# A fused recurrence, expert attention and spectral mix on one core: scores issued two chunks ahead, the next batch's first clamps moved, the weights' high parts reordered

## The chip, the cores and the metric

The kernel runs on one core of one Trainium2 chip. The metric is device time in microseconds (us) of one execution; lower is better. Before the change the median of three runs is 546.18 us (546.09 to 546.51).

## The reference, cut to what matters

Three layers follow each other, for 4 batches of 768 tokens, all in float32. Only the first and the start of the second lie around the change.

```python
# 1: gated linear recurrence, 8 heads of 48
f = 1.0 / (1.0 + np.exp(-f_logit))
for t in range(S):
    state = f[:, :, t, :, None] * state + np.einsum('bhd,bhe->bhde', k[:, :, t], v[:, :, t])
    y[:, :, t] = np.einsum('bhd,bhde->bhe', q[:, :, t], state)
# 2: x = y with the heads side by side (768 x 384); 4 experts of width 64, the best 2 per token
logits = x @ w_gate
for e in range(E):
    q, k, v = x @ wq[e], x @ wk[e], x @ wv[e]
    a = softmax(where(causal, -1e9, scale * q @ k.T))
    out += mask_e[..., None] * w_e * (a @ v @ wo[e])
# 3: theta = x @ w_theta; x cos(theta), x sin(theta) mixed over tokens by two 768 x 768 matrices,
#    added to x, then u + relu(u @ w_ch)
```

## The kernel before, in words

Every engine has a program of its own, written out by hand, and semaphores tie them together: an instruction waits until a counter has a value, and an engine never passes its own waiting instruction. So the order of calls in the text of each engine is the order on the chip. Batches are 0 to 3; `it` is the batch in the code.

**The gates.** The sigmoid of the gate logits is taken as a logarithm, `ln(1 + exp(-x))`: VectorE clamps one head pair (`clamp_gates`, L969), ScalarE takes Exp (L598) and Ln (L603), VectorE scans (`scan`, L975), ScalarE makes the decays from the scan (L607, L622, L627), and GpSimd scales q and k with them (L529, L532). This is done for batch b+1 while batch b is worked on. For batch 0 it is done first thing, in three parts of 256 tokens.

**The recurrence** is computed in 6 chunks c of 128 tokens. In a chunk TensorE has four blocks of work:

- scores of chunk c (`scores`, L1403): k times q of 8 heads, 16 weight loads, on 64 x 128 parts of the array, two row halves in turn; into one of two PSUM buffers, c % 2;
- turn_k (L1458): k of a chunk turned for the state's increment, on 64 x 128 parts too, 8 loads and products 48 wide;
- increments (L1476): turned k times v, on 128 x 64 parts, 16 loads, products 48 wide;
- outputs (L1495 with the masked scores, L1501 with the state): on 128 x 32 parts, 56 loads, products 128 wide.

VectorE masks the scores (`mask`, L1103; its output Am shares memory with `probT` and is shown under that name), which needs scores(c) and, as Am has two buffers, the outputs of chunk c-2. Then it adds the increment to the state (L1121) and decays it (L1125). ScalarE copies the turned k (L765) and the outputs (L776, L777). In the order before, chunk c of TensorE's loop is scores(c+1), turn_k(c+1), increments(c), outputs(c). VectorE's loop is mask(c+1), then the state of c.

**The ring.** When VectorE has made the low part of x for chunk n (`x_low`, L1044; ScalarE made the high part), TensorE multiplies x by the value and gate weights (6 products, n = 0 to 5), then by the query and key weights (8 products), each as high*high + high*low + low*high (L1385 to L1387). VectorE copies the values out (L1180), computes the routing (L1200 to L1220) and makes the low parts of q and k (`qk_l`, L1241). The query and key products need the low parts of their weights, which in batch 0 GpSimd makes (L535), once all of x's low parts and all four clamps are done.

**The attention.** TensorE's first expert scores (L1545) stand in front of the last two ring products and wait for the fourth `qk_l`. From there, VectorE's maxima (L1230), ScalarE's exponentials (L834) and TensorE's transposes (L1450) and products (L1608) hand work to each other. Layer 3 (4 batches after all four of layer 2) follows; it is nearly all TensorE.

The code below has the waits of each.

Of the kernel before, what the change touches and what calls it, by code (L numbers as in the profile page):

```python
# [26 lines left out]
NT = T // P  # L27
# [194 lines left out]
def build(nc, fT, qT, kT, vT, v, wq, wk, wv, w_gate, wo, woT, w_theta, w_tok, w_ch, out, slow_x):  # L222
    with ExitStack() as ctx:
# [268 lines left out]
        def _(pool):  # L492
# [46 lines left out]
            pool.wait_ge(w_hi, 1)  # L539
# [54 lines left out]
        def _(act):  # L594
# [152 lines left out]
            for it in range(B):  # L747
# [11 lines left out]
                def recurrence_copies():  # L759
                    for c in range(NT):  # L760
# [17 lines left out]
                        if it < 1:  # L778
                            if c == 2:
                                grow_first(2)  # L780
                            elif c == 3:
                                act.wait_ge(w_in[0], 32)
                                hi(wqk_h[:, :, :], staged(W_QK, 1536), w_hi)
                                act.wait_ge(w_in[1], 32)
                                hi(wvg_h[:, :, 0:256], wv_raw, w_hi)
                                hi(wvg_h[:, :, 256:260], graw[:, :, :], w_hi)
                            elif c == NT - 2:
                                for n in range(NT - 2):
                                    x_high(n)
                            elif c == NT - 1:  # L790
                                x_high(NT - 2)
                                exp_gates(1, (0, 1))
# [44 lines left out]
                for n in range(FIRST_QK, RING):  # L837
                    if n == FIRST_QK:
# [5 lines left out]
                        if it < 1:  # L844
                            log_gates(1, (0, 1))
                            exp_gates(1, (2, 3))
                            log_gates(1, (2, 3))
                            grow(1, 0)
                        elif it < B - 1:
                            if it == 1:  # L850
                                late_weights()
                            grow(it + 1, 1)
# [104 lines left out]
        def _(dve):  # L957
# [139 lines left out]
            for it in range(B):  # L1097
# [13 lines left out]
                for c in range(NT - 1):  # L1111
# [17 lines left out]
                    if it < 1:  # L1129
# [6 lines left out]
                        elif c == NT - 3:  # L1136
                            clamp_gates(1, 0)
                            clamp_gates(1, 1)
                        elif c == NT - 2:
                            dve.wait_ge(w_hi, 3)  # L1140
# [34 lines left out]
                if it < 1:  # L1175
                    clamp_gates(1, 2)
                    clamp_gates(1, 3)
# [204 lines left out]
        def _(pe):  # L1382
# [63 lines left out]
            for it in range(B):  # L1446
# [70 lines left out]
                for c in range(1, NT):  # L1517
                    if it < 1 and c == 2:
                        pe.wait_ge(v_in, 16)
                    if c + 1 < NT:  # L1520
                        scores(it, c + 1)
                        if c + 2 < NT:
                            turn_k(c + 1)
                        increments(c)
                    outputs(c)
# [255 lines left out]
```

## Time and profile before

| what | value |
|---|---|
| median of three runs | 546.18 us |
| the profiled execution's own time | 545.76 us |
| its span, first to last instruction | 544.0 us |
| TensorE matmul busy | 520.8 us (96%) |
| TensorE weight load busy | 487.3 us (90%) |
| VectorE busy | 384.8 us (71%) |
| ScalarE busy | 286.0 us (53%) |
| GpSimd busy | 133.7 us (25%) |
| granted TensorE clock | full in all 40 slices |

The time is read against the span: 1.8 us of the execution's own time lie outside it. PE is TensorE's products and PEld its weight loads; for the small products of the recurrence the loads are the better clock, since a load's start is recorded and the end of a product is modelled. A bracket at a row's end gives the idle time in front of it and what ended it; "issue" means that nothing the profile shows ended it. The three stretches of recurrence of batches 1 to 3 lie at 92, 162.6 and 233 us, that of batch 0 at 14.8 to 39.6 us.

### The profile page before, as it was taken

The numbers are of one execution on the slowest core, as the hardware profiler recorded it, in microseconds if no ns is written. First come the engines' busy times: TensorE is split into PE (matmuls) and PEld (weight loads), VectorE is DVE, ScalarE is ACT, GpSimd is POOL, SyncE is SP. The second block draws the span as 40 slices with busy tenths as digits, with TensorE's granted clock in tenths as the row PEclk, the third lists the DMA queues.
The fourth block names the chain that finished last, engine by engine and source line by source line (L and its number), as shares of the span: only waits on it lengthen the run. The fifth ranks groups of instructions, "written<-read, shape, count | busy, mean of one in ns | idle before, by whom it ended". The sixth has DMA issues, their size and how long they took to land.

```text
span 544.0 us, 14180 instructions
## 1 busy us (share of the span) xinstructions
PE 520.8 (96%) x6012; PEld 487.3 (90%) x6012; DVE 384.8 (71%) x698; ACT 286.0 (53%) x591; POOL 133.7 (25%) x89
## 2 busy tenths in 40 slices
PE   3999999999999999999999999999999999999997
PEld 1679778997889988899978899999999999999997
DVE  5989988898797977765877698585347654574434
ACT  5767687656976459642587574343234333333311
POOL 2005064065500054100214257112211212022110
PEclk9999999999999999999999999999999999999999
DMA  8958022072210620003500000311030201220032
GB/s 279 339 195 332 1 61 61 4 284 82 60 30 4 220 118 2 2 4 132 220 1 2 1 2 0 88 46 43 1 82 20 74 0 40 51 87 1 0 88 87
DMA packets 24832, 42.74 MB, mean 79 GB/s; under 512 B 3264, under 2 KB 15552, under 8 KB 24384
## 3 DMA queue, kind: packets, MB, share of 16 engines
q1 hardware_dynamic: 24768, 41.83, 23.5%
q8 instruction: 47, 0.77, 0.6%
q14 instruction: 17, 0.14, 0.1%
HBM read 32.25 MB, written 4.72 MB: 68 GB/s over the span
## 4 chain that ended last, share of the span: by engine, by line
PE 81%; DVE 7%; ACT 7%; issue 2%; DMA 1%; SPq 1%; DVEq 0%; ACTq 0%
PE bank L1385 18%; PE bank L1387 18%; PE bank L1386 18%; PE bank L1403 5%; ACT prob L834 5%; PE bank L1608 5%; PE bank L1545 4%; PE bank L1495 4%; PE bank L1450 2%; PE bank L1501 2%; PE bank L1476 2%; DVE nmax L1230 1%; DVE gate L975 1%; DMA OT<-w_theta 1%; DVE probT L1250 1%
## 5 line engine op out<-in xcount | busy, mean ns | idle before, releaser
L1385 PE MATMUL bank<-wt_h,z_h 128*128 128x384 f32 x288 | 97.0, 337 | 0.0
L1387 PE MATMUL bank<-wt_h,z_l 128*128 128x384 f32 x288 | 96.7, 336 | 0.0
L1386 PE MATMUL bank<-wt_l,z_h 128*128 128x384 f32 x288 | 96.4, 335 | 0.0
L834 ACT ACTIVATE prob<-bank,nmax 128x384 f32<-128x384 f32 (+5 forms) x96 | 60.3, 638 | 21.1 <-DVE nmax L1230 21.1
L589 POOL TENSOR_TENSOR trig<-trig,x 128x768 f32<-128x768 f32 x18 | 33.5, 1860 | 142.3 <-ACT trig L708 142.3
L1230 DVE TENSOR_REDUCE nmax<-bank 128x1 f32<-128x384 f32 (+5 forms) x96 | 54.9, 616 | 10.3 <-PE bank L1551 5.2
L1059 DVE TENSOR_SCALAR turns<-bank 128x384 int32<-128x384 f32 x22 | 12.2, 554 | 68.1 <-PE bank L1387 68.1
L1385 PEld LDWEIGHTS bank<-wt_h,z_h 128*128 128x128 f32 x288 | 54.0, 188 | 0.3 <-issue 0.3
L1387 PEld LDWEIGHTS bank<-wt_h,z_l 128*128 128x128 f32 x288 | 54.1, 188 | 0.0
L1386 PEld LDWEIGHTS bank<-wt_l,z_h 128*128 128x128 f32 x288 | 54.0, 187 | 0.0
L1608 PE MATMUL bank<-probT,Vm 128*64 128x128 f32 x672 | 42.0, 276 | 0.7 <-DVE probT L1250 0.2
L700 ACT COPY x<-bank 128x384 f32<-128x384 f32 x24 | 11.5, 478 | 55.2 <-PE bank L1387 55.2
L1608 PEld LDWEIGHTS bank<-probT,Vm 128*64 128x64 f32 x672 | 36.2, 137 | 2.9 <-DVE probT L1250 1.4
L1103 DVE TENSOR_TENSOR probT<-bank,keep 128x1024 f32<-128x1024 f32 x24 | 29.3, 1221 | 10.8 <-PE bank L1403 10.7
L1495 PE MATMUL bank<-probT,V 128*32 128x128 f32 x768 | 35.8, 275 | 0.7 <-issue 0.7
L1545 PE MATMUL bank<-qk_h 64*128 64x512 f32 (+3 forms) x128 | 26.2, 407 | 7.6 <-ACT prob L834 5.8
L705 ACT ACTIVATE trig<-r 128x384 f32<-128x384 f32 x22 | 11.6, 527 | 41.6 <-DVE r L1071 41.6
L1385 PE MATMUL bank<-xT_h,wqk_h 128*128 128x384 f32 x96 | 32.9, 343 | 0.0
L1386 PE MATMUL bank<-xT_l,wqk_h 128*128 128x384 f32 x96 | 32.4, 338 | 0.0
L1387 PE MATMUL bank<-xT_h,wqk_l 128*128 128x384 f32 x96 | 32.4, 337 | 0.0
L1250 DVE COPY probT<-bank 128x896 f32<-128x896 f32 x24 | 26.0, 1085 | 7.8 <-PE bank L1450 7.8
L1403 PE MATMUL bank<-q,k 64*128 64x128 f32 x384 | 29.8, 291 | 1.4 <-issue 1.4
(179 smaller groups left out, 1371.9 us busy)
## 6 DMA issues: line engine op xcount, KB each, us to landing
gate<-fT SPq DMA_DIRECT2D x12, 384.0 KB, 3.2
q<-qT SPq DMA_DIRECT2D x12, 384.0 KB, 5.4
k<-kT SPq DMA_DIRECT2D x12, 384.0 KB, 6.3
wt_raw<-w_tok SPq DMA_DIRECT2D x6, 768.0 KB, 8.8
uT<-xb SPq DMA_DIRECT2D x64, 72.0 KB, 2.1
out<-uT SPq DMA_DIRECT2D x24, 192.0 KB, 2.3
V<-v SPq DMA_DIRECT2D x3, 1344.0 KB, 11.1
gate<-fT SPq DMA_DIRECT2D x3, 512.0 KB, 5.6
```

Of the source, the lines that this page charges most:

```text
L589: nc.gpsimd.tensor_tensor(trig[:, s % 2, :, :], trig[:, s % 2, :, :], x2[:, s:s + 1, :].broadcast_to([P, 2, D]), ALU.mult).then_inc(z_made, 1)
L834: nc.scalar.activation(prob[:, m % 2, r, at], bank[r][:, at], ACT.Exp, bias=nmax[:, m, k:k + 1], accum_out=den[:, m // 2, which, e:e + 1]) ...
L1103: nc.vector.tensor_tensor(Am[:, c % 2, :, :], bank[c % 2][:, :].rearrange("p (h t) -> p h t", h=H), keep[:, None, :].broadcast_to([P, H, P ...
L1230: nc.vector.tensor_reduce(nmax[:, m, k:k + 1], bank[r][:, columns_of(m, which)], X, ALU.max, negate=True).then_inc(max_done, 1)
L1250: nc.vector.tensor_copy(probT[:, m % 2, 1, :].rearrange("p (c h q) -> p h c q", h=2, q=64), turned(m, 1)).then_inc(pt_copied[0], 1)
L1385: nc.tensor.matmul(o, a_h, b_h, start=start, stop=False)
L1386: nc.tensor.matmul(o, a_h, b_l, start=False, stop=False)
L1387: return nc.tensor.matmul(o, a_l, b_h, start=False, stop=stop)
L1403: mm = nc.tensor.matmul(bank[c % 2][:, slot(h):slot(h) + P], k[r:r + 64, h // 2, at], q[r:r + 64, h // 2, at], start=True, stop=True)
L1495: mm = nc.tensor.matmul(dst, V[:, c, at:at + BLOCK], Am[:, c % 2, slot(h) // P, :], start=n == 0, stop=c == 0 and n + 1 == len(parts), ski ...
L1545: mm = nc.tensor.matmul(bank[r][:, lo_:hi_], x[rows, a, queries], y[rows, 2 + a, keys], start=fresh_bank and n == 0, stop=False, skip_grou ...
L1608: mm = nc.tensor.matmul(ps(values_bank(m))[64 * r:64 * r + 64, at], Vm[:, s, e * ED:(e + 1) * ED], probT[:, m % 2, r, n * P:(n + 1) * P], ...
```

## The change

It has four parts. (1) TensorE: in the recurrence the scores run two chunks ahead: the chunk loop becomes turn_k(c+1), increments(c), scores(c+2), outputs(c), with scores(2) still in front at c = 1. In batch 0 scores(4) stays behind the outputs of chunk 2, since its q and k are scaled late. (2) VectorE: the clamps of batch 1 for pairs 0 and 1 leave the recurrence of batch 0 (c = 3), those for pairs 2 and 3 leave the place behind the low parts, and all four now stand behind x_low(1) to x_low(4). (3) ScalarE: the exponentials of batch 1's pairs 0 and 1 leave the last chunk of batch 0's recurrence and stand after it. (4) ScalarE makes the high part of the query and key weights after those of the value weights; the counts of `w_hi` that others wait for follow.

```diff
-            pool.wait_ge(w_hi, 1)
+            pool.wait_ge(w_hi, 3)
...
                                 act.wait_ge(w_in[0], 32)
-                                hi(wqk_h[:, :, :], staged(W_QK, 1536), w_hi)
                                 act.wait_ge(w_in[1], 32)
                                 hi(wvg_h[:, :, 0:256], wv_raw, w_hi)
                                 hi(wvg_h[:, :, 256:260], graw[:, :, :], w_hi)
+                                hi(wqk_h[:, :, :], staged(W_QK, 1536), w_hi)
...
                             elif c == NT - 1:
                                 x_high(NT - 2)
-                                exp_gates(1, (0, 1))
...
                         if it < 1:
-                            log_gates(1, (0, 1))
-                            exp_gates(1, (2, 3))
-                            log_gates(1, (2, 3))
+                            for pairs in ((0, 1), (2, 3)):
+                                exp_gates(1, pairs)
+                                log_gates(1, pairs)
                             grow(1, 0)
...
-                        elif c == NT - 3:
-                            clamp_gates(1, 0)
-                            clamp_gates(1, 1)
                         elif c == NT - 2:
-                            dve.wait_ge(w_hi, 3)
+                            dve.wait_ge(w_hi, 2)
...
                 for n in range(NT):
                     x_low(n)
-                if it < 1:
-                    clamp_gates(1, 2)
-                    clamp_gates(1, 3)
+                    if it < 1 and 1 <= n < NT - 1:
+                        clamp_gates(1, n - 1)
...
+                    late = it < 1 and c + 2 == NT - 2
                     if c + 1 < NT:
-                        scores(it, c + 1)
+                        if c == 1 or it < 1 and c + 1 == NT - 2:
+                            scores(it, c + 1)
                         if c + 2 < NT:
                             turn_k(c + 1)
                         increments(c)
+                        if c + 2 < NT and not late:
+                            scores(it, c + 2)
                     outputs(c)
```

Above that loop the changed file drops comment lines, so its numbers are 5 lower: its scores are L1398, turn_k L1453, increments L1471, outputs L1490 and L1496.

This is how TensorE's program stands in batch 1, from the scores of chunk 3 to the outputs of chunk 3 (before). Each row is one block; the outputs of a chunk are some 14 rows, of which the first two stand here.

```order
L1403 MATMUL bank<-q,k 128x128 x8
L1458 MATMUL bank<-ident,k 128x48 x8
L1476 MATMUL bank<-V,kTs 48x48 x8
L1495 MATMUL bank<-probT,V 32x128 x4
L1501 MATMUL bank<-q,S 32x128
...
L1403 MATMUL bank<-q,k 128x128 x8
L1458 MATMUL bank<-ident,k 128x48 x8
L1476 MATMUL bank<-V,kTs 48x48 x8
L1495 MATMUL bank<-probT,V 32x128 x4
```

The same place in the changed program, from the increments of chunk 1 on:

```order
L1471 MATMUL bank<-V,kTs 48x48 x8
L1398 MATMUL bank<-q,k 128x128 x8
L1490 MATMUL bank<-probT,V 32x128 x4
L1496 MATMUL bank<-q,S 32x128
...
L1453 MATMUL bank<-ident,k 128x48 x8
L1471 MATMUL bank<-V,kTs 48x48 x8
L1398 MATMUL bank<-q,k 128x128 x8
L1490 MATMUL bank<-probT,V 32x128 x4
```

The scores, which stood between outputs and turn_k, now stand between increments and outputs. The number of instructions is the same.

VectorE in batch 0, from the first low part of x on, before:

```order
L1044 TENSOR_TENSOR xT_l<-xt,xT_h 128x3x128 x6
L969 TENSOR_SCALAR gate<-gate,floor 128x768 x2
L1180 COPY Vm<-bank 128x260 x4
L975 SCALAR_TENSOR_TENSOR gate<-fresh,gate 128x768
L1180 COPY Vm<-bank 128x260
```

and in the changed program:

```order
L1043 TENSOR_TENSOR xT_l<-xt,xT_h 128x3x128 x2
L968 TENSOR_SCALAR gate<-gate,floor 128x768
L1043 TENSOR_TENSOR xT_l<-xt,xT_h 128x3x128
L968 TENSOR_SCALAR gate<-gate,floor 128x768
L1043 TENSOR_TENSOR xT_l<-xt,xT_h 128x3x128
L968 TENSOR_SCALAR gate<-gate,floor 128x768
L1043 TENSOR_TENSOR xT_l<-xt,xT_h 128x3x128
L968 TENSOR_SCALAR gate<-gate,floor 128x768
L1043 TENSOR_TENSOR xT_l<-xt,xT_h 128x3x128
L1175 COPY Vm<-bank 128x260 x4
```

Four clamps now stand between the first low part and the first copy of values, where two stood; the other two came from the recurrence, ahead of this piece.

## Rows read from the trace of the kernel before

**Rows 1.** Stages: busy time of each engine in batch 1's recurrence.
```profile
core 0: us, PE busy (x) PEld busy (x) DVE busy (x) ACT busy (x) POOL busy (x), PEclk, DMA share, GB/s
92.00:110.50 18.50, 18.50 (x516) 16.66 (x512) 15.35 (x24) 12.89 (x25) 0.38 (x1) 1.00 0.02 6
```

**Rows 2.** Timeline, TensorE's weight loads, batch 1 (start, us, instruction, [idle before]).
```profile
98.64 0.97 PEld L1403 LDWEIGHTS bank<-q,k 64*128 64x128 f32 x16 [0.20 <-issue]
99.52 0.39 PEld L1458 LDWEIGHTS bank<-ident,k 48*128 48x128 f32 x8
99.96 0.44 PEld L1476 LDWEIGHTS bank<-V,kTs 128*48 128x48 f32 x16
100.46 0.16 PEld L1495 LDWEIGHTS bank<-probT,V 128*32 128x32 f32 x8
...
102.12 0.97 PEld L1403 LDWEIGHTS bank<-q,k 64*128 64x128 f32 x16 [0.20 <-issue]
...
105.61 0.97 PEld L1403 LDWEIGHTS bank<-q,k 64*128 64x128 f32 x16 [0.20 <-issue]
106.70 0.44 PEld L1476 LDWEIGHTS bank<-V,kTs 128*48 128x48 f32 x16
...
109.15 0.11 PEld L1501 LDWEIGHTS bank<-q,S 128*32 128x32 f32 x1 [0.27 <-DVE S L1125]
...
110.60 0.19 PEld L1385 LDWEIGHTS bank<-wvg_h,xT_h 128*128 128x128 f32 x1 [0.20 <-issue]
```

**Rows 3.** Timeline, VectorE, end of batch 1's recurrence.
```profile
106.82 1.23 DVE L1103 TENSOR_TENSOR probT<-bank,keep 128x1024 f32<-128x1024 f32 x1 [1.14 <-PE bank L1403]
...
109.89 2.88 DVE L1044 TENSOR_TENSOR xT_l<-xt,xT_h 128x384 fp32r<-128x384 f32 x6
```

**Rows 4.** The chain that ended last, after batch 1's recurrence.
```profile
110.33 2.42 DVE xT_l L1044 x5
```

**Rows 5.** Timeline, TensorE's weight loads, batch 0.
```profile
27.34 0.37 PEld L1458 LDWEIGHTS bank<-ident,k 48*128 48x128 f32 x8 [1.61 <-issue]
27.76 0.44 PEld L1476 LDWEIGHTS bank<-V,kTs 128*48 128x48 f32 x16
...
31.75 0.14 PEld L1495 LDWEIGHTS bank<-probT,V 128*32 128x32 f32 x5
32.85 0.11 PEld L1495 LDWEIGHTS bank<-probT,V 128*32 128x32 f32 x2 [0.96 <-issue]
...
34.50 0.97 PEld L1403 LDWEIGHTS bank<-q,k 64*128 64x128 f32 x16 [0.20 <-issue]
35.60 0.44 PEld L1476 LDWEIGHTS bank<-V,kTs 128*48 128x48 f32 x16
...
39.89 0.19 PEld L1385 LDWEIGHTS bank<-wvg_h,xT_h 128*128 128x128 f32 x1 [0.59 <-issue]
```

**Rows 6.** DMA queues from 24 to 33 us: packets, MB, share of 16 engines.
```profile
q8 instruction: 2, 0.03, 1.4%
```

**Rows 7.** Timeline, VectorE, batch 0.
```profile
33.88 0.62 DVE L969 TENSOR_SCALAR gate<-gate,floor 128x768 f32<-128x768 f32 x1 [0.47 <-DMA gate<-fT]
...
35.72 1.23 DVE L1103 TENSOR_TENSOR probT<-bank,keep 128x1024 f32<-128x1024 f32 x1 [0.19 <-PE bank L1403]
...
39.22 2.90 DVE L1044 TENSOR_TENSOR xT_l<-xt,xT_h 128x384 fp32r<-128x384 f32 x6 [0.28 <-ACT xT_h L757]
42.04 1.14 DVE L969 TENSOR_SCALAR gate<-gate,floor 128x768 f32<-128x768 f32 x2
...
44.55 0.43 DVE L1180 COPY Vm<-bank 128x260 f32<-128x260 f32 x1 [0.36 <-PE bank L1387]
44.90 2.09 DVE L975 TENSOR_TENSOR_SCAN gate<-fresh,gate 128x768 f32<-128x768 f32 x1
...
53.61 2.41 DVE L1241 SCALAR_TENSOR_TENSOR qk_l<-bank,qk_h 128x384 fp32r<-128x384 f32 x5
```

**Rows 8.** Timeline, GpSimd and ScalarE, batch 0.
```profile
38.83 1.57 ACT L598 ACTIVATE gate<-gate 128x768 f32<-128x768 f32 x2
...
43.37 6.85 POOL L535 TENSOR_TENSOR wqk_l<-OT,wqk_h 128x384 fp32r<-128x384 f32 x4 [14.45 <-DVE gate L969]
```

**Rows 9.** Timeline, TensorE's weight loads, first expert scores of batch 0.
```profile
56.11 0.19 PEld L1545 LDWEIGHTS bank<-qk_h 64*128 64x128 f32 x2 [0.25 <-DVE qk_l L1241]
```

## The prediction

> **What bounds the kernel now.** I read the page first: TensorE is busy nearly all the time, so a change pays only where TensorE waits or where its own work gets shorter. Then the stages: in batch 1's recurrence its products cover 18.50 of 18.50 us [rows 1]. Busy is not yet full speed, so I went to the weight loads in order of time [rows 2], where the reader should look at starts. From the scores of one chunk (98.64) to those of the next (102.12) it is 3.48 us: scores to turn_k 0.88, turn_k to increments 0.44, increments to outputs 0.50, outputs to scores 1.66. In none of these is there a wait for another engine. The only one in the whole recurrence is 0.27 us for the last state [rows 2]. Batches 2 and 3 show the same starts to 0.02 us. So what the change wants to take off the path, the wait of outputs for masked scores, is not there in three batches of four.
>
> Behind a recurrence the chain that ended last goes through VectorE's low parts and its backlog [rows 4]. VectorE itself idles 1.14 us before its last mask, waiting for scores(5), and is then busy up to the low parts [rows 3]. So it starts later whenever TensorE's recurrence ends later, and nothing swallows the delay.
>
> Batch 0 differs. There are two pauses of TensorE, 1.61 and 0.96 us, that no engine explains [rows 5]. Counted in TensorE's program they stand exactly 256 instructions apart, and in the same stretch the queue that carries instructions moved two packets [rows 6], while the 16 DMA engines were full of inputs. I take both as instructions that came late: then they belong to a place in the stream, not to a piece of work. At the end of that recurrence TensorE waits 0.59 us for VectorE [rows 5].
>
> **Part 1, scores ahead, batches 1 to 3.** All work is kept; what changes is the neighbours. Scores and turn_k use the array in the same 64 x 128 parts, and turn_k's loads start 0.88 us after the scores', before their last load is done. Where scores are followed by another shape, increments after scores(5), it is 1.09 us (105.61 to 106.70) [rows 2]. In the new order all three moved blocks are followed by outputs, another shape (128 x 32). I take 1.09 for each. Per batch two of them lose the cheap neighbour: 2 x (1.09 - 0.88) = +0.42. Increments before scores I price as increments before outputs, 0.50, and outputs before turn_k as outputs before scores, 1.66; these stay. A turn_k that starts afresh took 0.42 to the increments in batch 0 (27.34 to 27.76) [rows 5] against 0.44: -0.04 for two. **Per batch +0.38, for three batches +1.14 us.** Bounds: nothing, if outputs can follow scores as turn_k does; 0.15 more per block, if scores idle as long behind increments as behind outputs (0.44 of loads and 0.20 [rows 2], 0.64 against 0.50), for nine blocks.
>
> The 0.27 us wait stays. Before, mask(5) starts when scores(5) end, just as increments(4) begin (106.70, 106.82) [rows 2, 3]. After, mask(5) has its scores early but still needs the outputs of chunk 3, whose last product again ends as increments(4) begin. Mask, sum and decay then race the same outputs(4).
>
> The Trainium skill (TensorEngine Tiling (Array Packing), Key Properties) says that changing the tiling mode drains TensorE, and it speaks against this change, which turns three changes of shape per chunk into four. This trace agrees where products 128 wide are in flight (0.20, and 1.09 against 0.88) and not where they are 48 wide: turn_k to increments shows no idle time. By the page, every change drains, scores behind increments too; that is the upper bound above, and the sum would be 9 x 0.15 = 1.35 us higher.
>
> **Part 1, batch 0.** Only scores(3) and scores(5) move. The first pause lies one instruction before the end of scores(3). In the new stream that place is just behind the last product of outputs(1), so the outputs are counted as done before it, and VectorE's and ScalarE's work on q and k for chunk 4 keeps its time. I leave it at 1.61. Everything before the second pause again fits in front of 32.85. Before, 51 of 56 loads of outputs(3), then all of scores(5) lay between the pause and increments(4): 32.85 to 35.60 [rows 5]. After, the pause falls after 6 of the 16 loads of scores(5). What remains is some 0.7 us of them and 1.67 of outputs(3): 32.85 + 0.7 + 1.67 = 35.2. So 0.40 us are won, since scores use the time of the pause. mask(5) (35.72) moves to 35.3, and with it the first low part (39.22 to 38.8) and the ring (39.89 to 39.5) [rows 5, 7].
>
> The Trainium skill (Runtime: NRT & Kernel Launch, Instruction fetch mechanics) says instructions are refilled in blocks of 16 KiB, 256 instructions, with a cost that is "mostly hidden". The 256 agree with this trace; "hidden" does not hold in batch 0, where 1.61 and 0.96 us show. Were it hidden and the pauses due to the work, the sum would lose the 0.40.
>
> **Part 2, the clamps.** In the old place two of them cost nothing: VectorE waited around them (33.88) [rows 7]. In the new place VectorE has no slack: from 39.22 to the fifth `qk_l` it idles once, 0.36 us before the fourth copy [rows 7]. Two clamps are 1.14 less 0.08 of overlap, 1.06 us. Starting 0.40 earlier, filling the 0.36: 1.06 - 0.40 - 0.36 = **+0.30** for everything from the scan at 44.90 on. Who waits? Low part n gets behind by up to three clamps, 1.6 us, but the ring takes about 1.1 us a product and a low part 0.47, so x_low(n) still lands some 0.8 us early. GpSimd starts behind the last low part instead of the last clamp: 38.8 + 2.8 + 2.1 + 0.2 = 43.9 or 44.0 against 43.37 [rows 8], 1.71 us a part, first part at 45.7, second at 47.4; TensorE wants them at 39.5 + 6.6 = 46.1 and 1.6 later, 47.7. Thin, 0.3 us, but covered. The first expert scores want the fourth `qk_l`: 53.61 + 0.57 + 3 x 0.46 = 55.56, after 55.86, seen by TensorE at 55.92. TensorE itself would be there at 56.11 - 0.40 = 55.71 [rows 9]. **So 0.19 us of the 0.40 come through.** What follows is a chain of all three engines, and moves as one.
>
> **Parts 3 and 4.** ScalarE's two exponentials (1.57 us) [rows 8] leave the front of the last copy of x and wait for the new clamps, done at 40.4 and 41.4; two more activations of 0.8 and the first logarithm is there at 43.0, the scan needs it at 45.2. The value weights' high part comes 1.5 us earlier, but VectorE takes it behind the last state either way. Both nothing; if ScalarE were 2.2 us later it would show in the scan one to one.
>
> **Sum** against the profiled execution's 545.76: +1.14 - 0.19 = +0.95, 546.7. The median of the runs lies 0.42 above that execution: 546.18 + 0.95 = **547.1 us**. A measurement of this kernel tells about 0.2%, 1.09 us, from no change, so this sits just inside it.
>
> **The rivals.**
>
> - *Shape is free (546.0, chance 0.17).* Outputs follow scores as cheaply as turn_k does; then only batch 0's -0.19 is left. For: 128 x 32 parts could be loaded one by one. Against: the only change of shape after scores, 106.70, costs the 0.21.
> - *VectorE or GpSimd late in batch 0 (547.9, 0.16).* The clamps among the low parts delay the ring, or GpSimd's parts miss TensorE by a few tenths, or the second pause grows and the 0.40 is lost: +1.14 + 0.6. For: margins of 0.3 us. It decides from 0.15 us of extra delay on, when the sum passes 1.09.
> - *Every change drains (548.5, 0.07).* Scores behind increments idle a full 0.20: 0.64 - 0.50 = 0.14 to 0.15 in nine blocks, 1.35 on top of 547.1. Against: increments to outputs, also a change, shows 0.50 with 0.44 of loads.
> - *The gaps are waits (faster, about 544.0, 0.10).* The 0.20 before each scores block is the wait for the mask and not a drain. Then moving scores behind increments hides it: nine blocks and two in batch 0, 11 x 0.20 = 2.2 us off, and no 0.21 added: 546.2 - 2.2. It decides for faster once 0.10 of the 0.20 is such a wait and the 0.21 falls away. Against: the same 0.20 stands before the ring at 110.60, where no scores are involved [rows 2].
>
> **How the numbers follow.** My forecast has 0.50, its own range is 546.7 to 547.6: about 0.31 of it below 547.27 and 0.19 above. Faster 0.11 (the last rival and 0.01 of a larger gain in batch 0). Slower: 0.19 + 0.16 + 0.07, less a little where the late rival stays small: 0.41. Same: 0.48. The range 545.4 to 548.1 holds the forecast, the free shape and the late rival, and leaves the two outer ones.
>
> **What would show it.** Scores to outputs at 1.09 us in the loads of batches 1 to 3, and recurrences 0.4 us longer from first scores to ring. The 0.27 wait still there. In batch 0 a pause inside scores(5) after six loads, increments(4) near 35.2, the ring near 39.5, the first `qk_l` at 53.9, expert scores at 55.9. I am wrong if scores to outputs takes 0.9, if the pauses sit elsewhere or have other lengths, or if the ring of batch 0 shows gaps.

## The result: 2.3 us slower

| what | before | changed |
|---|---|---|
| median of the runs | 546.10 us (545.51 to 546.51, 6 runs) | 548.42 us (548.12 to 548.93, 6 runs) |
| ratio to before, 95% interval | | 1.0046 (1.0033 to 1.0059) |
| span of the profiled execution | 544.0 us | 546.4 us |

The change makes the kernel slower by 0.46%, more than the 0.2% that a measurement tells from no change. The forecast was 547.1, its range ended at 548.1, and the time lies 0.3 us above that.

The first place to look is where the difference builds up. These are the starts of the ring and of the first expert scores in each batch, read from TensorE's weight loads in both traces:

| batch | ring before | ring changed | difference | expert scores before | changed | difference |
|---|---|---|---|---|---|---|
| 0 | 39.89 | 39.47 | -0.42 | 56.11 | 56.24 | +0.13 |
| 1 | 110.60 | 111.48 | +0.88 | 126.84 | 127.69 | +0.85 |
| 2 | 181.13 | 182.76 | +1.63 | 197.36 | 198.97 | +1.61 |
| 3 | 251.66 | 254.01 | +2.35 | 272.04 | 274.39 | +2.35 |

So each recurrence of batches 1 to 3 is 0.72 to 0.74 us longer (the forecast had 0.38), batch 0 gives +0.15 at its end (forecast -0.19), and nothing behind the last recurrence adds or takes anything. 3 x 0.73 + 0.15 = 2.34 us, which is the difference of the last row and, to 0.1, that of the spans. These are two single executions. Where batch 0 begins differs between executions (see the experiments), so its row is worth less than the other three.

TensorE's weight loads in batch 1 of the changed kernel (start, us, instruction, idle before), to be laid beside [rows 2]:

```profile
103.51 0.33 PEld L1453 LDWEIGHTS bank<-ident,k 48*128 48x128 f32 x8 [0.20 <-issue]
103.89 0.44 PEld L1471 LDWEIGHTS bank<-V,kTs 128*48 128x48 f32 x16
104.39 0.97 PEld L1398 LDWEIGHTS bank<-q,k 64*128 64x128 f32 x16
105.48 0.16 PEld L1490 LDWEIGHTS bank<-probT,V 128*32 128x32 f32 x8
...
107.14 0.44 PEld L1471 LDWEIGHTS bank<-V,kTs 128*48 128x48 f32 x16 [0.20 <-issue]
108.25 0.19 PEld L1490 LDWEIGHTS bank<-probT,V 128*32 128x32 f32 x8 [0.67 <-issue]
...
111.48 0.19 PEld L1380 LDWEIGHTS bank<-wvg_h,xT_h 128*128 128x128 f32 x1 [0.20 <-issue]
```

Scores (104.39) to outputs (105.48) is the 1.09 of the forecast, turn_k afresh to increments 0.38 where it had 0.42. The new thing is 0.67 us of idle loads before outputs(4), and the 0.27 before the last state is gone. The row says "issue", so it names nobody. The chain that ended last does, in the same place (start, us, what):

```profile
107.28 0.48 ACT xT_h L776
107.76 0.39 ACT xt L777
108.15 0.14 issue
108.29 0.43 PE bank L1490 x8
```

The path leaves TensorE here for ScalarE's two copies of the outputs of chunk 3. The cost groups of the page say it for the whole program (busy, mean ns, idle before and its releaser):

```profile
L1490 PE MATMUL bank<-probT,V 128*32 128x128 f32 x768 | 35.1, 275 | 2.3 <-ACT xt L777 1.9
L1490 PEld LDWEIGHTS bank<-probT,V 128*32 128x32 f32 x768 | 29.1, 109 | 4.6 <-issue 2.5
```

ScalarE's own timeline shows that the copies themselves are prompt, as they were before. First the changed kernel, then the same two copies in the kernel before, where outputs(4) began only at 107.19:

```profile
107.28 0.48 ACT L776 CAST xT_h<-bank 128x384 fp32r<-128x384 f32 x1 [1.66 <-PE bank L1496]
107.66 0.48 ACT L777 COPY xt<-bank 128x384 f32<-128x384 f32 x1
```

```profile
105.75 0.48 ACT L776 CAST xT_h<-bank 128x384 fp32r<-128x384 f32 x1 [1.51 <-PE bank L1501]
106.12 0.48 ACT L777 COPY xt<-bank 128x384 f32<-128x384 f32 x1
```

Outputs of chunks 1 to 4 all go to PSUM bank 4 (`out_bank`), so outputs(4) wait until both copies of outputs(3) are out. That is 1.1 us after outputs(3) have ended and increments(4) begun (107.14 to 108.25). Before, scores(5) and increments(4) stood between the two outputs, 1.09 + 0.49 = 1.58 us. Now only the increments do, 0.49.

Batch 0 shows the same wait with one copy instead of two. There ScalarE makes the high part later, so only L777 stands between outputs(3) and outputs(4), and these begin 0.73 us after the increments (35.08 to 35.81 in the rows of batch 0 below).

The sum of one recurrence, from the loads of both traces: two scores blocks at 1.09 instead of 0.89, +0.40; two turn_k at 0.38 instead of 0.44, -0.12; increments(4) to outputs(4) 1.11 instead of 0.49, +0.62; outputs(4) and (5) 3.23 instead of 3.41, -0.18, since the state is now in time. Together +0.72.

Batch 0, TensorE's loads, to be laid beside [rows 5]:

```profile
27.02 0.35 PEld L1453 LDWEIGHTS bank<-ident,k 48*128 48x128 f32 x8 [1.75 <-issue]
...
31.41 0.52 PEld L1398 LDWEIGHTS bank<-q,k 64*128 64x128 f32 x6
32.55 0.74 PEld L1398 LDWEIGHTS bank<-q,k 64*128 64x128 f32 x10 [0.63 <-issue]
...
35.08 0.44 PEld L1471 LDWEIGHTS bank<-V,kTs 128*48 128x48 f32 x16 [0.20 <-issue]
35.81 0.19 PEld L1490 LDWEIGHTS bank<-probT,V 128*32 128x32 f32 x8 [0.29 <-issue]
...
37.32 0.11 PEld L1490 LDWEIGHTS bank<-probT,V 128*32 128x32 f32 x2 [0.24 <-issue]
...
39.47 0.19 PEld L1380 LDWEIGHTS bank<-wvg_h,xT_h 128*128 128x128 f32 x1 [0.26 <-issue]
...
56.24 0.19 PEld L1545 LDWEIGHTS bank<-qk_h 64*128 64x128 f32 x2 [0.80 <-DVE qk_l L1236]
```

The first pause stands behind outputs(1), the second inside scores(5) after six loads. There is a small third one, 44 loads into outputs(4), again 256 instructions on. Neither this pause nor the wait for the copy reaches the ring. It starts 0.11 us after the first low part of x is finished (38.80 + 0.56 to 39.47), as it did before (39.22 + 0.56 to 39.89). VectorE in the same batch, to be laid beside [rows 7]:

```profile
35.29 1.23 DVE L1102 TENSOR_TENSOR probT<-bank,keep 128x1024 f32<-128x1024 f32 x1 [2.15 <-PE bank L1496]
...
38.80 1.03 DVE L1043 TENSOR_TENSOR xT_l<-xt,xT_h 128x384 fp32r<-128x384 f32 x2 [0.27 <-ACT xt L777]
...
43.74 1.43 DVE L1175 COPY Vm<-bank 128x260 f32<-128x260 f32 x4
45.08 2.51 DVE L974 TENSOR_TENSOR_SCAN gate<-fresh,gate 128x768 f32<-128x768 f32 x1
47.52 0.40 DVE L1175 COPY Vm<-bank 128x260 f32<-128x260 f32 x1
47.84 2.19 DVE L974 TENSOR_TENSOR_SCAN gate<-fresh,gate 128x768 f32<-128x768 f32 x1
```

The first scan starts 0.12 before its forecast of 45.2 but takes 2.51 us, where it took 2.09. GpSimd, beside [rows 8]:

```profile
43.98 6.86 POOL L535 TENSOR_TENSOR wqk_l<-OT,wqk_h 128x384 fp32r<-128x384 f32 x4 [15.46 <-DVE xT_l L1043]
```

### The profile page after: what moved, and what is told of

The parts are those of the page before. It is cut to its first block, busy times and chain, and to the rows that moved or that the text cites. A ratio compares the mean times of both kernels' runs of the same rounds, so it can differ in the third digit from the quotient of the medians.

```text
span 546.4 us, 14181 instructions
## 1 busy us (share of the span) xinstructions
PE 519.6 (95%) x6012; PEld 486.9 (89%) x6012; DVE 385.3 (71%) x698; ACT 285.6 (52%) x591; POOL 133.8 (24%) x89
## 4 chain that ended last, share of the span: by engine, by line
PE 76%; DVE 11%; ACT 9%; issue 2%; DMA 1%; DVEq 0%
PE bank L1380 18%; PE bank L1382 17%; PE bank L1381 17%; ACT prob L833 5%; PE bank L1608 5%; PE bank L1398 4%; PE bank L1545 4%; PE bank L1490 4%; DVE gate L974 2%; PE bank L1445 2%; PE bank L1496 2%; PE bank L1471 1%; DVE nmax L1225 1%; DVE qk_l L1236 1%; DVE probT L1245 1%
## 5 line engine op out<-in xcount | busy, mean ns | idle before, releaser
L1490 PE MATMUL bank<-probT,V 128*32 128x128 f32 x768 | 35.1, 275 | 2.3 <-ACT xt L777 1.9
L1490 PEld LDWEIGHTS bank<-probT,V 128*32 128x32 f32 x768 | 29.1, 109 | 4.6 <-issue 2.5
```

The lines of the kernel that those rows point to most:

```text
L1490: mm = nc.tensor.matmul(dst, V[:, c, at:at + BLOCK], Am[:, c % 2, slot(h) // P, :], start=n == 0, stop=c == 0 and n + 1 == len(parts), ski ...
```

## The experiments

Before's median was 545.83, 545.64 and 545.81 us in the three sessions. "Ring" and "expert scores" below are starts in the trace, as differences to the trace of before. The start of an execution moves: in the kernels whose TensorE program is the same up to the first pause, that pause ends between 26.85 us (`clamps_back`) and 28.14 us (`first_only`). So batch 0 is judged by differences inside one trace.

### Each half alone

`scores_only` is the kernel before with the new order of scores and nothing else; `rest_only` is the changed kernel with the old order.

```diff
 # scores_only, against the kernel before
+                    late = it < 1 and c + 2 == NT - 2
                     if c + 1 < NT:
-                        scores(it, c + 1)
+                        if c == 1 or it < 1 and c + 1 == NT - 2:
+                            scores(it, c + 1)
...
                         increments(c)
+                        if c + 2 < NT and not late:
+                            scores(it, c + 2)
```

> The kernel before with the new order of scores alone (clamps, exponentials and weights' high parts as before). Theory A, from the trace of the changed kernel: in each of batches 1 to 3 outputs(4) waits about 0.67 us for ScalarE's copy of outputs(3), since scores(5) no longer stand between them, and the recurrence is 0.72 us longer; batch 0 wins the 0.4 us in front of its ring and keeps it, because no clamp was moved into VectorE's backlog. Sum: +3 x 0.72 - 0.4 = +1.8 us on the kernel before, about 547.9. Rival: the loss belongs to the clamps and VectorE's backlog in batch 0 and the new order is harmless: at most +0.4 us.

> The changed kernel with the old order of scores (so the clamps among the low parts, the exponentials behind the recurrence and the new order of weights' high parts are left). Theory A: batches 1 to 3 keep their 3.48 us per chunk and the single wait of 0.27 us; in batch 0 VectorE's backlog grows by two clamps less one idle 0.36 us, 0.7 us, and the fourth low part of q and k comes at about 56.3 to 56.6 us instead of 55.6, so the expert scores start 0.2 to 0.5 us late: +0.2 to +0.5 us, about 546.5. Rival: these parts carry the loss: +2 us. Rival: they cost nothing: 0.

`scores_only`: 548.31 us, ratio 1.0047 (1.0034 to 1.006). Recurrences +0.71 to +0.74 each, 0.67 before outputs(4), ring and expert scores of batch 0 both 0.33 earlier. `rest_only`: 546.16 us, ratio 1.0004 (0.9995 to 1.0012). Its recurrences keep 3.48 us a chunk and the 0.27 wait; its ring is 0.32 earlier, of which 0.25 are there when the first pause ends, its expert scores 0.23 later. So the recurrences of batches 1 to 3 make all that the measured times can tell, and the other parts cost some half a microsecond between the ring and the expert scores of batch 0.

The half microsecond is seen in traces alone. `scores_only` has a median 2.48 us above before, more than its three recurrences (2.2 us) and more than the 1.8 us that was expected with a gain in batch 0; its profiled execution, 547.58 us, was its fastest. By the medians it can't be told from the changed kernel.

### A bank of its own for outputs(4)

```diff
-    return 6 if c == NT - 1 else 4
+    return 6 if c == NT - 1 else 7 if c == NT - 2 else 4
...
-                    if 1 <= c < NT - 1:
+                    if 1 <= c < NT - 2:
```

The ring's product that uses bank 7 next waits for the copy of outputs(4) in its place.

> The changed kernel with outputs(4) written to a PSUM bank of their own (the one that the turned k of odd heads has left), so that they need not wait for the copy of outputs(3); the ring's fifth product, which uses that bank later, waits for the copy instead. Theory A: the 0.67 us wait of outputs(4) goes, the 0.27 us wait for the last state comes back, so each of batches 1 to 3 is 0.42 us shorter, and batch 0 stays: -1.3 us on the changed kernel, about 547.1. Rival: the wait was for something else (the mask, or instructions), and nothing changes.

547.36 us, ratio 1.0027 (1.0017 to 1.0037). Batch 1's loads:

```profile
107.03 0.44 PEld L1471 LDWEIGHTS bank<-V,kTs 128*48 128x48 f32 x16 [0.20 <-issue]
109.57 0.11 PEld L1496 LDWEIGHTS bank<-q,S 128*32 128x32 f32 x1 [0.36 <-DVE S L1124]
111.02 0.19 PEld L1380 LDWEIGHTS bank<-wvg_h,xT_h 128*128 128x128 f32 x1 [0.20 <-issue]
```

The wait before outputs(4) is gone and the one for the state is back. From first scores to ring a recurrence takes 18.91 us against 18.53 before, +0.38 in each of the three batches, which is the forecast's 0.38; from ring to ring a batch adds 0.35. In batch 0 the increments are again followed by outputs(4) after 0.50 us (35.04 to 35.54). With a bank of their own for outputs(4) half of each recurrence's loss goes: the wait for the copy is shown to be that half.

### Scores(5) back behind the outputs

```diff
-                    late = it < 1 and c + 2 == NT - 2
+                    ahead_by_two = c + 2 < NT - 1 and not (it < 1 and c + 2 == NT - 2)
...
-                        if c == 1 or it < 1 and c + 1 == NT - 2:
+                        if c == 1 or it < 1 and c + 1 == NT - 2 or c + 1 == NT - 1:
                             scores(it, c + 1)
...
-                        if c + 2 < NT and not late:
+                        if ahead_by_two:
```

> The changed kernel with scores(5) back in front of increments(4); scores(3), and from batch 1 on scores(4), stay ahead. Theory A: scores(5) again cover ScalarE's copy of outputs(3), the 0.67 us wait goes and 0.27 us for the state comes back: each of batches 1 to 3 is 0.42 us shorter, as with a bank of its own; batch 0 loses the 0.4 us that scores(5) won inside the pause for instructions, of which VectorE's backlog lets none through, or makes them late by as much: -0.9 to -1.3 us on the changed kernel, 547.1 to 547.5. Rival: each block of scores ahead costs the same and the last is not special: -0.3 us at most.

547.86 us, ratio 1.0036 (1.0023 to 1.0049), and 0.53 to 0.57 a batch. The expectation missed: the wait moved one chunk up instead of going.

```profile
104.94 0.19 PEld L1490 LDWEIGHTS bank<-probT,V 128*32 128x32 f32 x8 [0.29 <-issue]
...
110.18 0.11 PEld L1496 LDWEIGHTS bank<-q,S 128*32 128x32 f32 x1 [0.27 <-DVE S L1124]
```

Now outputs(3) have only turn_k(4) and increments(3) between them and outputs(2), 0.38 + 0.49 = 0.87 us where the copies need 1.11. So 0.24 is waited for, and the sum comes out again: +0.40 - 0.12 + 0.24 = 0.52, where a recurrence measures 19.08 to 19.09 us against 18.53. Whatever stands between two outputs has to cover the copies of the first.

### Keeping turn_k behind the scores

From c = 2 on the order is increments(c), scores(c+2), turn_k(c+1), outputs(c), with the bank of `own_bank`. Scores still run two chunks ahead, but their neighbour is the block of their own shape.

> The changed kernel with outputs(4) in a bank of their own, and turn_k put behind the scores in each chunk: chunk 1 is scores(2), scores(3), turn_k(2), increments(1), outputs(1), later ones are increments(c), scores(c+2), turn_k(c+1), outputs(c). Scores stay two chunks ahead, but every block of them is followed by a block on the same 64 x 128 parts. Theory A (what the move of scores costs, besides the copy wait, is the change of shape behind them): scores to turn_k 0.88 us again, turn_k to outputs 0.44, so a chunk takes 3.48 us as before and the recurrence of batches 1 to 3 is 0.0 to 0.2 us shorter than before; 1.1 us less than the changed kernel with its own bank alone, about 546.2. Rival (being ahead costs by itself, through PSUM or the masks): no better than that kernel, 547.3.

545.77 us, ratio 1.0000 (0.9991 to 1.0009).

```profile
100.33 0.97 PEld L1398 LDWEIGHTS bank<-q,k 64*128 64x128 f32 x16
101.22 0.38 PEld L1453 LDWEIGHTS bank<-ident,k 48*128 48x128 f32 x8
101.65 0.16 PEld L1490 LDWEIGHTS bank<-probT,V 128*32 128x32 f32 x8
...
103.32 0.44 PEld L1471 LDWEIGHTS bank<-V,kTs 128*48 128x48 f32 x16 [0.20 <-issue]
```

Scores to turn_k is 0.89 again, turn_k to outputs 0.43, and one recurrence is 18.43 us against 18.53 before. The 0.20 after the outputs stays and now stands before the increments: it belongs to leaving the products 128 wide, whoever follows. So both terms of the loss are removed by construction, the price of the neighbour by order and the copy by bank, and scores two chunks ahead are worth 0.1 us a recurrence by themselves in these batches, which the times can't tell from nothing.

### Only batch 0 ahead

```diff
+                    late = it < 1 and c + 2 == NT - 2
...
-                        scores(it, c + 1)
+                        if it >= 1 or c == 1 or c + 1 == NT - 2:
+                            scores(it, c + 1)
...
+                        if it < 1 and c + 2 < NT and not late:
+                            scores(it, c + 2)
```

> The kernel before with scores(3) and scores(5) ahead in batch 0 alone; clamps and all else as before. Theory A: scores(5) run inside the second pause for instructions, the ring of batch 0 and its expert scores start 0.3 to 0.4 us earlier, and everything behind moves by that: -0.35 us on the kernel before, 545.5 to 545.8. Rival (the gain is lost in VectorE's backlog): expert scores at 56.1 us as before, no difference.

545.96 us, ratio 1.0004 (0.9995 to 1.0013). In its trace ring and expert scores are 0.28 later, not earlier. The first pause ended 0.8 later, at 28.14 against 27.34; from there to the ring it is 12.04 us against 12.55. This is not the expected gain seen: the second pause is missing altogether in this trace, where TensorE came late to it, while `scores_only`, with the same order in batch 0 and a first pause that ended at 26.96, takes 12.60 us for the same stretch. The differences between executions are larger than the gain, and the times don't show it. Inconclusive.

### GpSimd earlier

`rest_only`, with GpSimd's low parts of the query and key weights waiting for the high parts alone:

```diff
             pool.wait_ge(w_hi, 3)
-            pool.wait_ge(x_lo, NT)
-            pool.wait_ge(clamped, gates(1, PAIRS))
```

> The changed kernel with the old order of scores (as in an earlier run), and GpSimd's low parts of the query and key weights no longer held until the low parts of x: they start when the high parts are made, at about 33 us. Theory B (VectorE's first two scans after the ring's start take 2.5 and 2.2 us instead of 1.75 because GpSimd subtracts beside them): both scans take 1.75 us, the fourth low part of q and k comes 1.1 us earlier, and the expert scores start at or before 55.8 us: -0.4 to -0.5 us on that run in the trace, if the masks of the recurrence, which now have GpSimd beside them, do not get longer. Rival: the scans stay at 2.2 to 2.5 us; the cause is another (reading the values' banks, ScalarE's logarithms).

547.58 us, ratio 1.0026 (0.9996 to 1.0056). The interval is wide and just takes in no change; the trace has its expert scores of batch 0 2.18 us later than before. It was to be faster and is not, but it tells what slows the scans. VectorE:

```profile
39.79 1.83 DVE L1041 TENSOR_TENSOR xT_l<-xt,xT_h 128x384 fp32r<-128x384 f32 x2
41.54 1.37 DVE L966 TENSOR_SCALAR gate<-gate,floor 128x768 f32<-128x768 f32 x1
42.84 1.35 DVE L1041 TENSOR_TENSOR xT_l<-xt,xT_h 128x384 fp32r<-128x384 f32 x1
44.11 0.61 DVE L966 TENSOR_SCALAR gate<-gate,floor 128x768 f32<-128x768 f32 x1
44.64 0.55 DVE L1041 TENSOR_TENSOR xT_l<-xt,xT_h 128x384 fp32r<-128x384 f32 x1
...
48.45 1.74 DVE L972 TENSOR_TENSOR_SCAN gate<-fresh,gate 128x768 f32<-128x768 f32 x1
```

and GpSimd beside it:

```profile
38.53 5.24 POOL L535 TENSOR_TENSOR wqk_l<-OT,wqk_h 128x384 fp32r<-128x384 f32 x4 [9.47 <-issue]
```

While GpSimd works (to 43.77) the second and the third low part take 1.36 and 1.35 us instead of 0.55 and a clamp 1.37 instead of 0.61; once it is done the scan takes 1.74 instead of 2.09 to 2.51. The collision had only been moved onto the low parts, which the ring waits for one by one: its loads idle 1.04 us before the first product and 1.43 until the third low part is there.

### The state before the mask

The kernel before with two blocks exchanged in the last step of a recurrence: TensorE does increments(4), scores(5), outputs(4), and VectorE takes the last state before the last mask.

> The kernel before with one change, in the last step of each recurrence: TensorE does increments(4), scores(5), outputs(4) instead of scores(5), increments(4), outputs(4), and VectorE adds and decays the last state before it masks scores(5) instead of behind it. Theory A: the 0.27 us wait for the last state is a race of mask, sum and decay (2.3 us) against increments(4) and outputs(4); with the state done while scores(5) run, only the mask is left behind them and outputs(5) find both ready. Each recurrence is 0.27 us shorter and VectorE gets to the low parts 0.5 us earlier: -0.8 to -1.5 us on the kernel before, about 545.0. Rival: outputs(5) then wait for the mask as long as they did for the state: no difference.

545.25 us, ratio 0.9990 (0.9981 to 1.0000). The recurrence of batch 1 is 18.45 us against 18.53, with 0.20 before outputs(5) in place of the 0.27. That is 0.08 where 0.27 was expected; the rival, that outputs(5) then wait for the mask instead, is most of the truth.

```profile
108.08 0.16 PEld L1498 LDWEIGHTS bank<-probT,V 128*32 128x32 f32 x8 [0.20 <-DVE probT L1103]
```

The rest of its 1.0 us of span (543.0) was there when batch 0 ended (its ring is 0.76 earlier), so most of it may be one execution's luck. It is the fastest version tried, and still inside the 0.2%.

### The clamps back, twice

`clamps_back` is the changed kernel, and `turn_no_clamps` the kernel `turn_behind`, each with the clamps and exponentials of batch 1 in their old places.

```diff
+                        elif c == NT - 3:
+                            clamp_gates(1, 0)
+                            clamp_gates(1, 1)
...
-                    if it < 1 and 1 <= n < NT - 1:
-                        clamp_gates(1, n - 1)
+                if it < 1:
+                    clamp_gates(1, 2)
+                    clamp_gates(1, 3)
```

> The changed kernel with the clamps and exponentials of batch 1 back in their old places, and nothing else undone. If part 2 costs some 0.5 us between ring and first expert scores of batch 0, these come at about 55.75 instead of 56.24 with the ring where it was (39.5), batches 1 to 3 keep their 0.72 to 0.74 us each, and the whole is 0.5 us below the changed kernel: ratio to before 1.0034 (1.0025 to 1.0045). If part 2 costs nothing, the ratio stays at 1.0046.

> The changed kernel with outputs(4) in a bank of its own, turn_k between scores and outputs, and the clamps and exponentials of batch 1 back in their old places. If the clamps among the low parts cost through VectorE's backlog and the longer first scan (0.3 to 0.5 us of batch 0), the first scan takes 2.1 to 2.25 us instead of 2.51, the first expert scores come 0.3 us earlier than in the kernel before (0.5 earlier than with the clamps moved), and the whole is 0.3 to 0.6 us below the kernel before: ratio 0.9990 (0.998 to 1.000). If the clamps cost nothing and the 0.3 us come from the order of TensorE, the expert scores stay 0.2 to 0.3 us late and the ratio is 1.0000.

`clamps_back`: 548.24 us, ratio 1.0043 (1.003 to 1.0057). `turn_no_clamps`: 545.67 us, ratio 0.9994 (0.9985 to 1.0003). From ring to expert scores both take 16.2 us, as before; the changed kernel, `rest_only`, `own_bank` and `turn_behind`, with the clamps among the low parts, take 16.75 to 16.77 (`last_late`, whose ring started 0.7 later, 16.43). This half of the expectation came true to 0.05 us. Both kernels also have ScalarE's exponentials back, so parts 2 and 3 are not told apart. Part 4 is still in both. But in `clamps_back` the ring started at 39.91 and not at 39.5, for the third late block of instructions, 0.24 in the changed kernel, was 1.34 us here:

```profile
34.49 0.44 PEld L1476 LDWEIGHTS bank<-V,kTs 128*48 128x48 f32 x16 [0.20 <-issue]
...
37.82 0.11 PEld L1495 LDWEIGHTS bank<-probT,V 128*32 128x32 f32 x2 [1.34 <-issue]
...
39.91 0.19 PEld L1385 LDWEIGHTS bank<-wvg_h,xT_h 128*128 128x128 f32 x1 [0.20 <-issue]
...
56.12 0.19 PEld L1550 LDWEIGHTS bank<-qk_h 64*128 64x128 f32 x2 [0.25 <-DVE qk_l L1241]
```

TensorE reached increments(4) 1.1 us before the kernel before did and then stood at the place of the next block. What batch 0 wins ahead of a block of instructions, the next block can take back. The ratio of 1.0034 that was expected was not met; its interval holds both that and the changed kernel's 1.0046, so the medians do not show what the clamps cost. Nor do they in `turn_no_clamps`, whose expert scores came 0.14 us later than before and not 0.3 earlier.

### Both small gains together

The kernel before, with the scores of batch 0 ahead (as `first_only`) and the end of `state_first` in batches 1 to 3.

> The kernel before with two orders: in batch 0 the scores run ahead as in the change, in batches 1 to 3 the last step is increments(4), scores(5), outputs(4), and VectorE takes the last state ahead of the last mask. The parts add: 0.3 to 0.4 us from the ring of batch 0, since scores(5) use the time of the second pause, and 0.08 in each later batch, in which a wait of 0.2 before outputs(5) is left of the 0.27 for the state. Ratio 0.9989 (0.998 to 1.000). If the ring's gain in batch 0 is taken up before the first expert scores, as it may be with VectorE's row of work behind it, 0.9996.

545.76 us, ratio 0.9999 (0.999 to 1.0008). The expert scores of batch 0 are 0.12 earlier, and each later batch adds 0.06 to 0.08, in all 0.33 us of span. The later batches are as expected; batch 0 gave a third of what was hoped, and less than its first pause ended early (27.17 against 27.34). The whole can't be told from no change.

## Why the prediction missed, step by step

**Part 1, batches 1 to 3, the price of the neighbour: right.** 1.09 where 1.09 was forecast; `own_bank` isolates it at +0.35 a batch, and `turn_behind` takes it away. That every change of shape drains is refuted: increments to scores is 0.50 in every trace (103.89 to 104.39). A free shape is refuted by the 1.09, and gaps that are waits for the mask by the 0.20, which stays behind the outputs and now stands before turn_k or the increments.

**"Increments before scores I price as increments before outputs, 0.50 ... Mask, sum and decay then race the same outputs(4)": the step that failed.** Increments(4) to outputs(4) stayed at 0.50 in the sum and measured 1.11. The step followed VectorE's race for the outputs and left out ScalarE's. Outputs(4) need the bank that outputs(3) filled, so they wait for two copies, which are done 1.1 us after outputs(3). Scores(5) had hidden that. The term missing from the sum is 0.62 for the wait less 0.18 that the state no longer costs, 0.44 a batch, less 0.08 because turn_k afresh was cheaper than taken. Three batches: 3 x 0.35 = 1.05 us. The 0.27 wait "stays" was wrong for the same reason. It would have stayed had the outputs not been late, as in `own_bank`, where it is 0.36.

**Part 1, batch 0: the places right, the 0.40 by luck.** The pauses are tied to the place in the program: behind outputs(1), after six loads of scores(5). Increments(4) at 35.08 (forecast 35.2) and the ring at 39.47 (39.5) also agree, but not for the reason given. The first pause, forecast to end at 27.34 as before, ended at 27.02, 0.32 earlier; from there to increments(4) the new order won only 0.20 (8.06 us against 8.26), and 0.10 of it was gone at the ring. `rest_only`, with the old order, had its ring at 39.57. With the new order in batch 0 (`scores_only`, `own_bank`, `first_only`, `clamps_back`, `state_ahead0`, the changed kernel) the ring starts anywhere from 39.43 to 40.18. So no run shows that the order wins the 0.40. The forecast also missed the third block, 256 further on, and the wait for the copy in batch 0. TensorE stood 0.24 us at each, and the ring's wait for VectorE took both in.

**Part 2, the clamps: the engines right, the term that decides wrong.** TensorE was ready for the expert scores at 39.47 + 16.22 = 55.69 (forecast 55.71), GpSimd started at 43.98 (43.9 or 44.0), the first scan at 45.08 (45.2). But the forecast let the scan keep its 2.09 us, and it took 2.51, so `qk_l` started at 54.23 and not 53.9, and the expert scores waited 0.55 us beyond the usual 0.25, not 0.2. The missing term is 0.34 us. It is the same late GpSimd that the forecast had computed: only its margin towards TensorE was looked at, not what it shares with VectorE. In all twelve kernels in which GpSimd starts behind the low parts, this one and the one before included, the first `qk_l` begins 10.24 to 10.26 us after GpSimd's first subtraction. GpSimd's 0.61 us of delay (43.37 to 43.98) was the price, and not the 0.30 that VectorE's own work added up to. The 1.71 us a part was a mean, too: the first two subtractions take 1.03 us each, so GpSimd's margin towards TensorE was wider than the 0.3 that the forecast saw.

**Parts 3 and 4: no wait in the trace names them.** Part 3 was never run without part 2. Part 4 is the only difference between `clamps_back` and `scores_only`: 548.24 us against 548.31, and 16.21 us against 16.22 from ring to expert scores. It costs nothing that shows.

The two misses, 1.05 and 0.34, on the forecast's 0.95 give 2.34, the 2.35 between the two traces. The 1.05 comes again in the traces of `scores_only` and `clamps_back` (19.25 us a recurrence in both). The 0.34 is seen in traces only, and that the sum closes to 0.01 owes something to the luck of the 0.32 above. Of the rivals, VectorE late in batch 0 came true with 0.34 of the 0.79 us that it was priced at. None held the wait for the copy.

## What to carry to other kernels

Before a block is moved from between two others, list every resource that both of them share, and price what the block was hiding: where a bank of PSUM has to be copied out first, the copies' time that is no longer covered becomes a wait (here 1.11 us less the 0.49 of the increments), and no row of the old trace shows it, as it was no wait there. When scores or the like are to run ahead, move them together with the neighbour of their own array shape. And where a step makes another engine start later, ask which memory or port it shares with the engine under discussion, not only who needs its result.

## What the runs showed of the hardware

**VectorE and GpSimd block each other for whole instructions.** GpSimd's four equal subtractions take 1.03 us while VectorE copies from PSUM and up to 2.48 beside its scans (changed kernel; count, shortest, median and longest in ns, first and last start):

```profile
L535 POOL TENSOR_TENSOR wqk_l<-OT,wqk_h x4: 1026/1746/2475, 44.0 to 48.4; 128x384 fp32r<-128x384 f32 x4
```

In the single instructions the first two take 1.03 and the others 2.48 and 2.46. The first scan takes from 2.09 to 2.52 us in the twelve kernels in which it meets these subtractions, and in all of them it ends 1.61 or 1.62 us after the end of GpSimd's second one: 45.37 and 46.99 before, 45.98 and 47.59 changed, 45.19 and 46.80 in `scores_only`, 45.76 and 47.37 in `clamps_back`. It fits a scan that waits for the running subtraction and then takes nearly its undisturbed 1.74; where it started makes no difference. The Trainium skill (SBUF — State Buffer, Who interferes with whom, and SBUF: two separate sides) says that a VectorE instruction with two inputs in SBUF contends with a GpSimd instruction that reads SBUF, and that whoever starts first has the shared ports for the whole instruction. The traces agree with both, by the scans' ends and by low parts of 0.55 us that take 1.35 in `pool_early`.

**Instructions can come late in the middle of a program.** In batch 0 TensorE pauses at instructions 450, 706 and 962 of its program (weight loads and products counted), whatever work stands there: 1.18 to 2.17 us at the first in the thirteen traces, up to 1.37 at the second and up to 1.34 at the third, and nothing at one or both of the later two in some. In the traces of before, changed and `clamps_back` a packet of the queue that carries instructions starts 2.2 to 2.6 us ahead of each pause's end. A load of inputs on the DMA engines is not needed for it: they were all but full ahead of the second pause of the kernel before (share 1.00 from 30 to 32.5 us), but 27% busy from 35 to 37.5 us in `clamps_back`, where the third pause took its 1.34. That an earlier arrival at a block's end only lengthens the next pause was seen once clearly (`clamps_back`); how much of it is chance from run to run, and what sets the length, stays open.
